# The main expert's two layers as three products of rounded parts, with the parts made in slots over x

## The reference

```python
h = x @ w_in                                   # 512 -> 2048
g = where(h >= 1, h, where(h <= -1, 0, (h + 1) ** 2 / 4))
x2 = g @ w_out                                 # 2048 -> 512
logits = x2 @ w_gate; expert_idx = argmax(logits); gate_w = softmax(logits)[expert_idx]
# each expert takes its first 288 tokens
y = maximum(x2[its tokens] @ w1[e], 0) @ w2[e] # 512 -> 1024 -> 512, float32
out[token] = gate_w * y                        # 0 where a token found no place
```

## Time and profile before

| | us |
|---|---|
| median of 3 runs | 319.81 (319.79 to 320.04) |
| the profiled execution | 322.16 |
| its span, first to last instruction | 320.4 |
| TensorE busy | 308.2 (96%) |
| VectorE, ScalarE, Pool busy | 206.9, 143.3, 145.9 |
| attention | 0 to about 113 |
| first block, chunks 0 to 3 | from about 101 (its first tiles stand between attention's last) to 253.5 |
| main expert and few tokens | 253.5 to 314 |

### The profile page before, as it was taken

One profiled execution on the slowest core, in us unless ns is written; L12 is line 12 of the kernel. 1 busy time (PEld: TensorE's weight loads), 2 busy tenths in 40 slices (PEclk: granted clock), 3 DMA queues, 4 the chain that ended last, 5 costly groups with the idle time before them and its releaser, 6 DMA issues.

```text
span 320.4 us, 7043 instructions
## 1 busy us (share of the span) xinstructions
PE 308.2 (96%) x2725; PEld 251.5 (79%) x2725; DVE 206.9 (65%) x540; ACT 143.3 (45%) x318; POOL 145.9 (46%) x170
## 2 busy tenths in 40 slices
PE   7999999999999999999999999999999999999991
PEld 6566766766768898888999989899898877756681
DVE  5899998999985566978856377467654623522300
ACT  1777875875974326455624244253434312002020
POOL 4777997998998000918830032402520070700301
PEclk9999999999999999999999999999999999999998
DMA  8988884852376400000004058420230291059930
GB/s 161 184 190 208 215 224 90 201 170 43 127 178 169 135 0 2 2 0 2 2 0 74 2 219 308 76 37 3 38 64 12 62 414 50 3 191 398 396 143 10
DMA packets 76056, 38.48 MB, mean 120 GB/s; under 512 B 67026, under 2 KB 67034, under 8 KB 74996
## 3 DMA queue, kind: packets, MB, share of 16 engines
q1 hardware_dynamic: 72580, 36.76, 40.7%
q10 hardware_dynamic: 2416, 0.59, 0.9%
q0 software_dynamic: 1024, 0.64, 0.7%
HBM read 32.66 MB, written 5.43 MB: 119 GB/s over the span
## 4 chain that ended last, share of the span: by engine, by line
PE 95%; DVE 2%; issue 1%; POOL 1%; ACT 0%; POOLq 0%; DVEq 0%
PE bank_a L1686 17%; PE bank_b L1686 15%; PE bank_out L1643 6%; PE bank_a L1544 5%; PE bank_pt L1596 5%; PE bank_b L1746 4%; PE bank_pt L1746 4%; PE bank_a L1620 3%; PE bank_b L1898 3%; PE bank_b L1907 3%; PE bank_a L1898 2%; PE bank_a L1907 2%; PE bank_b L1539 2%; PE bank_out L1719 2%; PE bank_out L1640 2%; PE bank_out L2018 2%
## 5 line engine op out<-in xcount | busy, mean ns | idle before, releaser
L677 POOL TENSOR_SCALAR prob<-prob,rl,gate_loc 128x512 f32<-128x512 f32 (+3 forms) x64 | 41.4, 662 | 12.0 <-DVE rl L1139 12.0
L1686 PE MATMUL bank_a<-x_hi,win_hi 128*128 128x288 f32 x128 | 39.2, 307 | 0.0
L1686 PE MATMUL bank_b<-x_hi,win_hi 128*128 128x288 f32 x128 | 38.1, 298 | 0.0
L1686 PE MATMUL bank_a<-x_lo,win_hi 128*128 128x288 f32 x128 | 37.8, 295 | 0.0
L1686 PE MATMUL bank_b<-x_lo,win_hi 128*128 128x288 f32 x128 | 37.8, 295 | 0.0
L1686 PE MATMUL bank_a<-x_hi,win_lo 128*128 128x288 f32 x128 | 37.7, 294 | 0.0
L1686 PE MATMUL bank_b<-x_hi,win_lo 128*128 128x288 f32 x128 | 37.6, 294 | 0.0
L918 ACT ACTIVATE g_raw<-bank_a,biases 128x576 f32<-128x576 f32 x16 | 11.9, 743 | 52.6 <-DVE sq L1213 52.6
L855 ACT ACTIVATE prob<-prob,negmax 128x512 f32<-128x512 f32 (+3 forms) x64 | 35.0, 550 | 0.8 <-DVE negmax L1089 0.8
L761 POOL DMA_INDIRECT few_d<-row,slot_l x12 | 12.7, 1059 | 49.4 <-DVE jobs_f L1363 38.2
L1219 DVE TENSOR_TENSOR g_raw<-g_raw,sq 128x576 f32<-128x576 f32 x32 | 31.4, 981 | 2.4 <-ACT sq L919 2.4
(11 more groups left out here) (300 smaller groups left out, 762.6 us busy)
## 6 DMA issues: line engine op xcount, KB each, us to landing
w_sb<-in_moe_w_dram SPq DMA_DIRECT2D x6, 2048.0 KB, 12.8
win_raw<-in_moe_w_in_dram SPq DMA_DIRECT2D x4, 1024.0 KB, 5.7
wout<-in_moe_w_out_dram SPq DMA_DIRECT2D x4, 1024.0 KB, 5.9
win_raw<-in_moe_w_in_dram SPq DMA_DIRECT2D x1, 4096.0 KB, 14.0
out_dram<-zero_row SPq DMA_DIRECT2D x8, 288.0 KB
x_d<-x_rows SPq DMA_DIRECT2D x32, 72.0 KB
v_sb<-in_v_dram SPq DMA_DIRECT2D x16, 128.0 KB, 2.5
qn<-in_q_dram SPq DMA_DIRECT2D x24, 72.0 KB, 4.9
```

The lines of the kernel that those rows point to most:

```text
L677: pool.tensor_scalar(prob[u][:, h, :], prob[u][:, h, :], rl[:, c:c + 1], gate_loc[:, 2 * j + h:2 * j + h + 1], ALU.mult, ALU.mult).then_in ...
L1686: last = pe.matmul(h_bank(d)[:, t, :], w[:, m, f:f + P], x[c % 2][:, m, :], start=(m == 0 and n == 0), stop=(m == KT - 1 and n == 2))
```

## The change

The main expert's layers become three products each. The parts of its weights are made in eight slots (`we_hi`, `we_lo`, 512 columns each), four of them over `xT` and four over the buffers of x's parts. Sixteen parts go through them: parts 0 to 7 are the column blocks of w1, parts 8 to 15 the row blocks of w2. ScalarE rounds them (`expert_hi`), six within chunk 3; Pool subtracts (`expert_lo`). The second layer has f outermost and m within. Activations get parts too: `x2_hi` and `x2_lo`, `h_hi` by ScalarE's relu, `h_lo` by VectorE. The stores into the large table move to the general path. `row`, `slot` and `slot_l` get a copy for each chunk. The buffers of expert 1's and 2's weights move, which makes the loads of expert 2 wait for the few tokens' hidden layer. Banks of the few tokens' work, and the order of VectorE's and TensorE's last steps, change with it.

```diff
-        w_at = (w_first_at, xT_at, win_at)
+        w_at = (w_first_at, win_at, win_lo_at)
+        slot_at = [xT_at + 8 * DM * n for n in range(4)] + [x_at + X_SIZE * n for n in (0, 2, 1, 3)]
...
 (SyncE)
             expert_weights(1, sp.value_load(jobs[0:1, 0, 1:2], min_val=0, max_val=E - 1))
+            sp.wait_ge(s_fh, 1)
             expert_weights(2, sp.value_load(jobs[0:1, 0, 2:3], min_val=0, max_val=E - 1))
...
 (Pool)
-                for r in range(NR):
-                    pool.indirect_dma_start(out=slots_d[:, :], ...).then_inc(s_scat, 16)
+            def expert_lo(i):
+                pool.wait_ge(s_ah, i + 1)
+                src = w1_sb[0][:, :, i * P:i * P + P] if i < ET else w2_sb[0][:, i - ET, :]...
+                pool.tensor_tensor(lo, src, hi, ALU.subtract).then_inc(s_al, 1)
             for c in range(1, NCH):
                 if c + 1 < NCH:
                     x_lo_part(c + 1)
+                else:
+                    for i in range(6):
+                        expert_lo(i)
                 scatter(c)
+            for i in range(6, ET + 5):
+                expert_lo(i)
             scatter(NCH)
+            for i in range(ET + 5, 2 * ET):
+                expert_lo(i)
...
 (ScalarE)
+            def x2_hi_part():
+                for n in range(2):
+                    act.wait_ge(s_xst[n], 16 * 4 * NPAIR // 2)
+                act.wait_ge(s_ye, KT)
+                act.activation(x2_hi[:, :, :], x2T[:, :, :], ACT.Copy).then_inc(s_xh, 1)
+            def expert_hi(i):
+                if i == 0:
+                    ...
+                if i in (4, 6):
+                    act.wait_ge(s_h, ND * (NCH - 1) if i == 4 else ND * NCH)
+                if i >= ET:
+                    act.wait_ge(s_eh, i - ET + 1)
+                act.activation(we_hi[i % ET]..., src, ACT.Copy).then_inc(s_ah, 1)
+                    if c == NCH - 1 and d == 4:
+                        x2_hi_part()
+                    if c == NCH - 1 and d in (3, 5, 6):
+                        for i in ((0, 1), (), (2, 3), (4, 5))[d - 3]:
+                            expert_hi(i)
-            hidden(0, True)
+            expert_hi(6)
+            expert_hi(7)
+            for f in range(ET):
+                act.wait_ge(s_eh, f + 1)
+                if f == 0:
+                    act.wait_ge(s_g, ND * NCH - 1)
+                act.activation(h_hi[:, f, :], e_bank(f)[:, 0:SLOTS], ACT.Relu).then_inc(s_ehe, 1)
+                expert_hi(ET + f)
+                if f == 4:
+                    exponentials(NCH)
...
 (VectorE)
-                if c > 1:
-                    dve.wait_ge(s_few, 16 * NR * (c - 1))
-                    dve.wait_ge(s_scat, 16 * NR * (c - 1))
+            def hidden_lo(f):
+                dve.wait_ge(s_ehe, f + 1)
+                dve.scalar_tensor_tensor(out=h_lo[:, f, :], in0=e_bank(f)[:, 0:SLOTS], scalar=0.0, in1=h_hi[:, f, :],
+                                         op0=ALU.max, op1=ALU.subtract).then_inc(s_hl, 1)
             chunks(dve, chunk)            # with x2_lo_part() in chunk 3, d = 5
+            hidden_lo(0)
+            hidden_lo(1)
             copy_lt(NCH)
+            hidden_lo(2)
             choose(NCH)
+            hidden_lo(3)
+            hidden_lo(4)
             place(NCH)
+            hidden_lo(5)
+            hidden_lo(6)
             rank_tokens(NCH)
+            hidden_lo(7)
...
 (TensorE)
-                    if c == NCH - 1 and d == ND - 1:
-                        logits(c, NQ - 2)
+            def main_first(f):
+                bank_read(f)
+                pe.wait_ge(s_al, f + 1)
+                if f > 3:
+                    pe.wait_ge(s_ehe, f - 3)
+                    pe.wait_ge(s_hl, f - 3)
+                for m in range(DT):
+                    for n, (w, x) in enumerate(((we_hi, x2_hi), (we_hi, x2_lo), (we_lo, x2_hi))):
+                        last = pe.matmul(e_bank(f)[:, 0:SLOTS], w[f][:, part], x[:, m, :], ...)
+                last.then_inc(s_eh, 1)
+            def main_second(f):
+                pe.wait_ge(s_al, ET + f + 1)
+                for m in range(DT):
+                    pe.wait_ge(s_hl, 5 + m if f == 0 else f + 1)
+                    for n, (w, x) in enumerate(((we_hi, h_hi), (we_hi, h_lo), (we_lo, h_hi))):
+                        last = pe.matmul(e_bank(m)[:, 0:SLOTS], w[f][:, part], x[:, f, :], ...)
-                if f == 1:
-                    logits(NCH - 1, NQ - 1)
+                if f < 2:
+                    logits(NCH - 1, NQ - 2 + f)
-            expert(0, bank_read, route_between, within_main)
+            for f in range(ET):
+                main_first(f)
+                route_between(f)
+            for f in range(ET):
+                main_second(f)
+                if f == 4:
+                    spread_list()
+                if f == 6:
+                    few_hidden()
+            few_turned()
+            expert_rows(0, range(2))
             ...                           # the few tokens' x2 (L1983), now into bank_o
+            expert_rows(0, range(2, slot_tiles))
```

More of the change, by code:

```diff
@@ L233, in build_program @@
         offset[0] = phase
+        y_row = [sb(f"y_row{r}", [ST, DM], F32)[0] for r in range(slot_tiles)]
         x2_few, _, _ = sb("x2_few", [P, DM_PART], F32)
@@ L429, in build_program, with jobs_of @@
         STATIC = 16 * slot_tiles
-        def jobs_of(eng, work):
+        def jobs_of(eng, work, first=None):
             eng.wait_ge(s_job, 2)
@@ L435, in jobs_of @@
             with eng.If(number > 0):
+                if first:
+                    first()
                 with eng.Fori(0, E) as n:
@@ L1335, in place @@
                 after(c, "slotf")
[L1336 to L1339 removed]
+                step(c, "slot", dve.tensor_tensor(slot[:, c - 1, :], slot_f, over, ALU.add))
                 dve.wait_ge(s_ex, c)
@@ L1888, in _, with expert @@
             chunks(pe, chunk)
-            def expert(J, ahead, between, within):
+            def expert(J):
                 for f in range(ET):
-                    ahead(f)
                     if f > 3:
@@ L1909, in expert, with expert_rows @@
                     last.then_inc(s_ey, 1)
-                    within(m)
-            def expert_rows(J):
+            def main_first(f):
[5 more added lines that the diff above has]
+                for m in range(DT):
+                    part = slice(m * P, m * P + P)
+                    for n, (w, x) in enumerate(((we_hi, x2_hi), (we_hi, x2_lo), (we_lo, x2_hi))):
+                        last = pe.matmul(e_bank(f)[:, 0:SLOTS], w[f][:, part], x[:, m, :],
+                                         start=(m == 0 and n == 0), stop=(m == DT - 1 and n == 2))
+                last.then_inc(s_eh, 1)
[3 more added lines that the diff above has]
+                    pe.wait_ge(s_hl, 5 + m if f == 0 else f + 1)
+                    part = slice(m * P, m * P + P)
+                    for n, (w, x) in enumerate(((we_hi, h_hi), (we_hi, h_lo), (we_lo, h_hi))):
+                        last = pe.matmul(e_bank(m)[:, 0:SLOTS], w[f][:, part], x[:, f, :],
+                                         start=(f == 0 and n == 0), stop=(f == ET - 1 and n == 2))
+                    if f == ET - 1:
+                        last.then_inc(s_ey, 1)
+            def expert_rows(J, tiles):
                 pe.wait_ge(s_eye, DT * (J + 1))
-                for r in range(slot_tiles):
+                for r in tiles:
                     for m in range(DT):
@@ L2059, in work @@
                 pe.wait_ge(s_ye, KT * (n + 2))
-                expert(n + 1, nothing, nothing, nothing)
-                expert_rows(n + 1)
+                expert(n + 1)
+                expert_rows(n + 1, range(slot_tiles))
             jobs_of(pe, work)
```

151 lines of the change are left out of this document (84 added, 67 removed).

## The result

The changed kernel takes 330.05 us, the median of 4 runs (328.86 to 331.14); the kernel before, run beside it on the same chip, takes 319.84 us (319.79 to 320.04). The ratio is 1.0317, 95% interval 1.0272 to 1.0363: some 10 us slower, where 1.9 us less were forecast. The profiled execution took 331.14 us with a span of 329.0. The four runs fall into two pairs, 2 us apart: about 331 us at a mean granted clock of 0.971, and about 329 us at 0.98; the profile is of the first pair.

A forecast was written before the change was run, and what follows sets the result against it. TensorE bound the kernel (95% of the chain). 6.9 us (6.3 products, 0.6 wait) leave its work, but G comes 1.4 us later and expert 2's weights end last: 1.9 us off 319.81 gives 317.9 us, range 314.4 to 320.6.

The forecast's parts named there:

- the tiny steps of routing: VectorE's last routing: steps reading two SBUF tiles, or such a tensor_scalar, wait for Pool's running subtraction, at most 1.3 us each.
- D: Rival: VectorE slows Pool's subtractions in turn; at 1.83 us each the time is 323.3 us; chance 0.12.
- G: Landing of the few tokens' gathered rows, where the first weights are issued: forecast 284.15, against 282.78 before.
- the fourth scatter: Pool's scatter behind the last placing, after the seven subtractions: forecast to start at 273.15.
- the gather: Pool's gather of the few tokens' rows: forecast at 281.0, against 279.62 before, 7.9 us behind the fourth scatter.
- From G to the end: Expert 2's weights end last: its w1 lands at G + 19.5, TensorE ends at G + 27.9, 1.9 us less than before.
- An f of three products: One step of the main expert's first layer on TensorE: 1.60 us instead of 2.0.
- The 0.6 us wait before the last logits: TensorE's wait for VectorE: gone, since the third quarter of the last logits moves behind the first f.
- ACT's roundings: Sixteen roundings at 0.63 us on ACT: two fit into each gap of chunk 3, costed at nothing.
- The third scatter: Pool's scatter of chunk 3: starts at 257.6 instead of 256.47, as the fifth subtraction makes a sum end 1.0 us later.
- rival C: The sum at 253.26 also gets in ahead of Pool's subtraction: G = 280.9, 314.7 us; chance 0.10.
- The 6.3 us that the products save: Main expert's layers on TensorE: 64 matmuls become 192 products, 25.6 us, 6.3 us less.

The follow-up runs named there:

- e8: The changed kernel with each of Pool's sixteen subtractions made to wait for the end of the one before it: 322.13 us, ratio 1.0054 to the kernel before.
- e3: The kernel before, with seven unused SBUF-reading subtractions added on Pool ahead of the fourth scatter: 330.98 us, ratio 1.0275.
- e9: The kernel before, with SyncE waiting for the few tokens' hidden layer ahead of expert 2's loads: 320.49 us, ratio 1.0002.
- e11: e5 with the main expert's row stores to the output held until expert 2's first matrix is in: 317.08 us, ratio 0.9904.
- e5: The changed kernel with ten of the sixteen subtractions (parts 6 to 15) on VectorE instead of Pool: 317.53 us, ratio 0.9918 to the kernel before.
- e12: e8 with 24 unused transposes in TensorE's idle time before expert 2's first layer: 319.62 us, ratio 0.9975 to the kernel before.
- e6: The changed kernel with seven subtractions (parts 6 to 12) on VectorE, the last three left on Pool: 321.59 us, ratio 1.0044 to the kernel before.
- e10: e5 with experts 0 and 1 of the few tokens finished before expert 2 is begun: 319.43 us, ratio 0.9965.

## Why the prediction was wrong

**The step that failed** is the price of "the tiny steps of routing" that "wait for the running subtraction each time", with "1.3 us (a whole subtraction) a step" as its upper end. That was no upper end. The rows it rested on cannot tell a subtraction from a row of them: one was a single instruction of 4.56 us, in the others Pool waited 0.30 us for its next part each time. In the change each of the parts 6 to 12 was rounded before Pool came to it, so Pool ran seven without a break, and one step paid 7.98 us. e8 puts the openings back and gives the forecast's own chain; e3 puts only the row of seven into the kernel before and gives the loss. The trace of before did show unbroken rows, at 130.93 and 144.22, and there a two-input step waited for one subtraction only; but those steps were wide. As the prediction itself says, the trace had no tiny two-input step under a subtraction. Carrying the price of the wide ones over to the tiny ones was the error; with no such row at hand the upper end was "the whole row", 7 x 1.30 = 9.1 us. The measured 330.05 us lies beyond every rival, D's 323.3 included.

**What it did to G.** Measured G is 7.3 us later than forecast: 5.1 at the fourth scatter (278.29 for 273.15), 2.3 between it and the gather (10.1 us for 7.9), where jobs_w is held for 4.27 us and the lists end behind the three subtractions, not before. Within the 5.1, the half clock behind 6.2 us of idle time adds about 2.5 us (3.09 + 2.69 for two f of 1.6 to 1.7).

**From G to the end**, a second error, which would have stood without the first: G + 31.8 for G + 27.9. Expert 2's first matrix lands at G + 21.1 instead of 19.5 (1.6 us; e9 gives 0.6 of this to SyncE's wait, e11 against e5 0.9 to the stores, which stand elsewhere against G than before). Of the other 2.3 us, 1.9 go with the clock: first layer 3.64 for 1.97, turns 1.22 for 1.0. The second layers' 5.84 for 5.42 are not the clock: they start when it is back at 1.00, and e5, at 1.00 throughout, has 5.84 too, but e12 5.42; why stays open. The forecast took these durations from a kernel whose TensorE did not wait there, and itself put a wait of 2 us in front of them; it became 4.6 us. Idle times of 4.6 us (the changed kernel here), 3.95 us (e8) and 2.74 us (e6) were followed by 0.50, those of 1.54 us (e12) and 2.08 us (e5) by 1.00.

**What held.** An f of three products takes 1.60 us where the clock is 1.00 and another f stands before it, in both layers: in e5 the chain has 0.78 to 0.80 us for nearly every half f of the second. Behind other work an f takes 1.69 to 1.79 us, which makes the first layer of e5 13.6 us, where 12.8 were counted. The 0.6 us wait before the last logits is gone. ACT's roundings fit into the gaps: chunk 3's last banks take 3.30 and 3.20 us for 24 products, as before. The third scatter starts at 256.54, where 257.6 was forecast, since the fifth subtraction did not hold the sum: the sum, at 252.71, took its usual 0.75 us and the subtraction, at 252.54, took 2.08. That was rival C's condition. In the row of seven a subtraction takes 1.25 us, so rival D, the slower side, had the right sign by the wrong mechanism: there VectorE does not slow Pool, Pool shuts VectorE out. Rival C said that G below 280 had no room on Pool; with the parts on VectorE (e5) G is 279.83 and the time 317.53 us beside 320.46 before, which is the gain forecast (1.9 us) or a little more, by another route. (The 6.3 us that the products save are 6.2 by the prediction's own rows; nothing hangs on it.)

## What to carry to other kernels

Before work is moved to Pool, look at which Vector instructions with two SBUF inputs, the smallest above all, can start while it runs. A tiny one is to be priced at all that is left of Pool's unbroken row, not at one instruction. Then break the row with a wait that is really waited, or put such work on the engine that would be shut out (0.68 us a part against 1.25 and a hold of 8). When a forecast lets TensorE wait several microseconds, price what comes behind the wait by rows at the lower clock too. The chain of waits does not give an engine's idle time; its list of waits does. A bound from rows is only a bound if the rows have the pattern of the change, the size of the steps included.

## What the runs showed of the hardware

- A Vector step of 96x24 or 1x64 elements with two SBUF inputs is held for the rest of an unbroken row of Pool's SBUF reads: 7.98 and 4.27 us. Six memsets of 0.1 us within the row do not end the hold (8.26 us). A semaphore wait of Pool on its own last instruction does (steps of 0.64 to 1.10 us) and costs the row 0.9 us.
- Steps of 128x288 and 128x576 with two SBUF inputs get in between two subtractions of such a row (1.30 us for a sum of 0.75), and the next subtraction then takes 1.51 to 1.83 us instead of 1.29.
- The same steps pass under memsets (0.16 us), and with one input in PSUM under subtractions (0.18 us); a tensor_scalar of 96x3 in SBUF is held by memsets for 3.90 us.
- Behind 6.2 us without a matmul TensorE had a granted clock of 0.50 for about 6 us, its lower level of 1.2 GHz, and an f took 3.09 us instead of 1.7. 24 transposes in an idle time of some 4 us took 0.8 points off the ratio.
- TensorE can stop with nothing to wait for in the profile: for 0.80 us in the kernel before, at 304.31, while some 390 GB/s of weights flow in, and for 1.89 us in e10, while the rate falls from 193 to 33 GB/s. What does this was not settled.
